# Value products as query x feature in a fused sink-window attention and two feed-forward layers

## The reference

```python
# q, k, v: 2 x 8 heads x 768 positions x 64, fp32
scores = q @ k.T / sqrt(64)
keep = (key < 4) | ((0 <= query - key) & (query - key < 128))
a = exp(where(keep, scores, -1e9) - rowmax)
a = a / (a.sum(-1) + 1e-9)
x = (a @ v)            # heads side by side: 1536 tokens x 512
h = x @ w_in;  x = max(0.01 * h, h) @ w_out        # 512 -> 2048 -> 512
h = x @ w_in2; y = (h * sigmoid(h)) @ w_out2       # 512 -> 2048 -> 512
```

## Time and profile before

| | us |
|---|---|
| median of three runs | 687.84 |
| the profiled execution | 690.34 |
| its span | 688.4 |
| PE busy | 634.6 |
| VectorE busy | 326.2 |
| ScalarE busy | 325.9 |
| GpSimd busy | 92.2 |

### The profile page before, as it was taken

How to read it: one execution, slowest core, us unless ns; L and a number is a source line. 1 busy time by engine, 2 the same in 40 slices (tenths; PEclk the granted TensorE clock), 3 DMA queues, 4 the chain that set the end, 5 groups by cost and what they waited for, 6 DMA issues and landing times.

```text
span 688.4 us, 9721 instructions
## 1 busy us (share of the span) xinstructions
PE 634.6 (92%) x3368; PEld 546.0 (79%) x3368; DVE 326.2 (47%) x780; ACT 325.9 (47%) x764; POOL 92.2 (13%) x117
## 2 busy tenths in 40 slices
PE   3649798979988999999999999999999999999997
PEld 3549798878887788888788888888888888888886
DVE  4786787746865666675322224333212322122321
ACT  5576677656765566664333336433323333223331
POOL 6341232222230322220000000000000000000000
PEclk9768999999999999999999999999999999999999
DMA  6643535413433213111002221323310112111001
GB/s 169 173 137 114 166 123 153 127 31 113 135 93 109 63 53 110 55 62 62 0 31 70 79 66 64 120 92 99 106 72 31 62 62 67 69 48 62 31 0 62
DMA packets 18096, 57.52 MB, mean 84 GB/s; under 512 B 2688, under 2 KB 2688, under 8 KB 18048
## 3 DMA queue, kind: packets, MB, share of 16 engines
q1 hardware_dynamic: 18048, 56.89, 26.9%
HBM read 53.74 MB, written 3.15 MB: 83 GB/s over the span
## 4 chain that ended last, share of the span: by engine, by line
PE 77%; DVE 10%; issue 5%; ACT 5%; DMA 1%; POOL 1%; SPq 0%; ACTq 0%; DVEq 0%; POOLq 0%
PE y_ps L841 34%; PE h_ps L810 33%; PE o_ps L774 3%; DVE sm L572 2%; PE y_ps L810 2%; PE t_ps L752 2%; PE s_ps L738 2%; DVE prob L646 2%; DVE x L593 1%; DMA qk_raw<-qk 1%; DVE win L599 1%; ACT pT L467 1%; DVE pT L582 1%; ACT q_st L447 1%; ACT win L479 1%
## 5 line engine op out<-in xcount | busy, mean ns | idle before, releaser
L810 PE MATMUL h_ps<-x,win 128*128 128x512 f32 (+1 forms) x1152 | 263.3, 374 | 6.1 <-DVE x L593 6.1
L810 PEld LDWEIGHTS h_ps<-x,win 128*128 128x128 f32 x1152 | 204.8, 190 | 42.4 <-issue 6.7
L610 DVE TENSOR_TENSOR g<-g_f,g 128x512 fp32r<-128x512 f32 (+1 forms) x112 | 72.4, 646 | 282.3 <-ACT g L494 282.3
L492 ACT ACTIVATE g_f<-h_ps 128x512 f32<-128x512 f32 (+1 forms) x96 | 53.9, 561 | 235.9 <-PE h_ps L810 235.6
L841 PE MATMUL y_ps<-g,wout 128*128 128x256 f32 (+1 forms) x768 | 153.6, 342 | 1.2 <-PE o_ps L774 0.9
L841 PE MATMUL y_ps<-wout,g 128*128 128x512 f32 x576 | 138.2, 389 | 0.0
L841 PEld LDWEIGHTS y_ps<-g,wout 128*128 128x128 f32 x768 | 120.9, 191 | 15.2 <-issue 1.5
L841 PEld LDWEIGHTS y_ps<-wout,g 128*128 128x128 f32 x576 | 108.1, 188 | 22.5
L436 ACT ACTIVATE prob<-sm,neg_max 128x260 f32<-128x260 f32 (+1 forms) x96 | 47.2, 491 | 65.5 <-DVE neg_max L572 64.8
L738 PE MATMUL s_ps<-k_hl,q_st 128*128 128x260 f32 (+1 forms) x162 | 35.8, 304 | 29.7 <-DVE neg_max L572 20.5
L599 DVE TENSOR_TENSOR win<-w_raw,win 128x512 fp32r<-128x512 f32 x72 | 53.5, 743 | 8.8 <-ACT win L479 8.4
(11 more groups left out here) (70 smaller groups left out, 428.0 us busy)
## 6 DMA issues: line engine op xcount, KB each, us to landing
w_raw<-w SPq DMA_DIRECT2D x72, 512.0 KB, 3.3
qk_raw<-qk SPq DMA_DIRECT2D x48, 260.0 KB, 4.7
v_raw<-vt SPq DMA_DIRECT2D x12, 256.0 KB, 2.6
y<-qk_raw SPq DMA_DIRECT2D x12, 256.0 KB, 2.2
vs_raw<-vsink SPq DMA_DIRECT2D x8, 8.0 KB, 2.3
```

The source lines that it names most:

```text
L492: nc.scalar.activation(g_f32[:, g_at(F)], h_of(F), func, alpha=slope)
L610: nc.vector.tensor_tensor(g[:, 1, g_at(F)], g_f32[:, g_at(F)], g[:, 0, g_at(F)].bitcast(F32), ALU.subtract).then_inc(g_ready, 1)
L810: ins = mm(h_of(F), win[:, split_slot[split_of[F]], wp, c * P:(c + 1) * P], x[:, xp, c, tokens(F)], start=(c == 0 and wp == HI and xp == H ...
```

## The change

- `weigh_values` swaps the operands: `pT` (128 keys x 128 queries of one head) is stationary and v moves with its 64 features. The result of a tile is query x feature for all 8 heads in one bank. `weigh_sinks` is one matmul of 512 columns for each tile.
- The probabilities are no longer scaled. `exp` collects the sums of a tile, `invert_sums` inverts 8 at a time, and a new `normalise(T)` multiplies the tile's result into `att` (128 x 512) in SBUF. Four transposes (job `"x"`) bring `att` to feature x query; `high` and `low` write it to `x`.
- `s_bank`: from slot 12 on the second score product of a slot gets a free bank of y (in slot 20, and from slot 36 on, `s_ps`), and stands behind the whole hidden step.
- `ticks_of`: two steps a slot for F = 0 to 13 (slots 11 to 17), then one. Step 32, the first wide one, moves from slot 35 to slot 36. The first two hidden steps move from the end of slot 10 into slot 11, behind the scores 22 and 23.
- ScalarE takes the hidden step ahead of the second exponential and the weight splits; the last transposes of tile T move into the middle of a hidden step in slot 4T + 6; SyncE issues the first two weight transfers before slot 0 and the next at slots 4 and 6; the sink values are stacked at slot 7 instead of 5; the zeroing of `prob_sink` is gone.

The matmul engine in a two-step slot: before, slot 13, `s_ps<-k_hl,q_st` are scores, `o_ps<-pT,v_hl` value products, `t_ps<-ident,prob` transposes.

The diff, cut to its core:

```diff
@@ the order
-    LAST = NPAIR + PAIRS
+    LAST = NPAIR + 4
-        n = (1, 1, 2)[(a - FS) % 3] if F < N_NARROW else 1
-        for _ in range(n):
+        for _ in range(2 if F < FT - 2 else 1):
-        lead = 0 if F == FT - 1 else 2 if F + 2 < N_NARROW else 1
+        lead = 2 if F + 2 < N_NARROW and F not in (FT - 2, FT - 1, FT) else 1
-    sinks_of = {2 * e + 3: e for e in range(NPAIR // 2) if has_sinks(e // 2)}
+    sinks_of = {PAIRS * T + 5: T for T in range(TILES) if has_sinks(T)}
+    x_of = {PAIRS * T + 6: T for T in range(TILES)}
@@ s_bank
+            a = n // 2
-            return (s_ps, y_ps[0], y_ps[1])[n % 3] if n < S_THREE else s_ps
+            if n < S_THREE:
+                return (s_ps, y_ps[0], y_ps[1])[n % 3]
+            if n % 2 == 0 or a == B1 or a >= B2:
+                return s_ps
+            return y_ps[2] if a < B1 else y_ps[0]
@@ sync
+            load_w(0)
+            load_w(1)
-                if 1 <= a <= RING:
-                    load_w(a - 1)
+                if a in (4, 6):
+                    load_w(a // 2)
@@ vector
-            def normalise(u):
-                W = width(u // PAIRS)
-                dve.wait_ge(exp_done, 2 * u + 2)
...
-                for i in range(2):
-                    a = prob[:, at + i, 0:W]
-                    nc.vector.tensor_scalar(a, a, row_inv[:, u % 2, 1, i:i + 1], None,
-                                            ALU.mult).then_inc(prob_ready, 1)
+            def invert_sums(T):
+                dve.wait_ge(exp_done, (T + 1) * H)
+                nc.vector.tensor_scalar_add(row_inv[:, 0, :], row_sum[:, T % 2, :], 1e-9).then_inc(norm_step, 1)
+                dve.wait_ge(norm_step, 2 * T + 1)
+                wait(dve, att_ready, T)
+                nc.vector.reciprocal(row_inv[:, 1, :], row_inv[:, 0, :]).then_inc(norm_step, 1)
+            def normalise(T):
+                dve.wait_ge(o_done, T + 1)
+                dve.wait_ge(norm_step, 2 * T + 2)
+                if T:
+                    dve.wait_ge(t_written, job["x", T - 1] + 1)
+                nc.vector.tensor_tensor(att[:, :].rearrange("p (h d) -> p h d", h=H),
+                                        o_bank(T)[:, :].rearrange("p (h d) -> p h d", h=H),
+                                        row_inv[:, 1, :].unsqueeze(2).to_broadcast([P, H, D]),
+                                        ALU.mult).then_inc(att_ready, 1)
@@ tensor
-                for s in slots:
-                    for vp, pp in PASSES:
-                        ins = mm(pair_out(u), v_hl[:, s, vp, p * P:(p + 1) * P],
-                                 pT[:, u % 2, pp, s * 2 * P:(s + 1) * 2 * P],
+                for i in range(2):
+                    h = 2 * p + i
+                    for s in slots:
+                        for pp, vp in PASSES:
+                            to = s * 2 * P + i * P
+                            ins = mm(o_bank(T)[:, h * D:(h + 1) * D], pT[:, u % 2, pp, to:to + P],
+                                     v_hl[:, s, vp, h * D:(h + 1) * D],
+                if a == FS:
+                    scores(2 * a + 1)
+                    for G in made_in[-1]:
+                        hidden(G, 0)
+                        hidden(G, 1)
                 for G in ahead[:1]:
                     hidden(G, 0)
-                if not head and a < NPAIR:
-                    scores(2 * a + 1)
+                if a in sinks_of:
+                    transposes("sinks", sinks_of[a])
+                if a in x_of and a <= NPAIR:
+                    transposes("pair", a - 1)
                 for n, G in enumerate(ahead):
                     if n:
                         hidden(G, 0)
                     hidden(G, 1)
+                if FS < a < NPAIR:
+                    scores(2 * a + 1)
```

More of the change, by code:

```diff
@@ L127, in sink_window_attention_two_ffn @@
             job["pair", a - 1] = len(job)
-    EARLY = next(a for a in range(LAST) if FT in ticks_of[a]) - 1
-    N_EARLY = job["pair", EARLY - 2] + 1
-    E_EARLY = 2 * NARROW // P
+        if a in x_of:
+            job["x", x_of[a]] = len(job)
+    N_EARLY = job["pair", FS - 2]
+    T_EARLY = NARROW // P
     S_FOUR, S_THREE = 2 * FS - 4, 2 * FS
+    B1, B2 = (next(a for a in range(LAST) if F in ticks_of[a]) for F in (FT, N_NARROW))
     with ExitStack() as ctx:
@@ L254, in width @@
             return P if T % TPB == 0 else PAN
[L256 to L260, removed]
         def j_split(T):
@@ L526, in _ @@
                     exp(2 * a)
-                    if head:
+                    if a <= FS:
                         exp(2 * a + 1)
-                if head and x_half is not None:
-                    high_x(x_half)
+                if a == FS:
+                    for G in made_in[-1]:
+                        take_hidden(G)
+                if a in sinks_of:
+                    high("sinks", sinks_of[a])
+                if not head and a in x_of and a <= NPAIR:
+                    high("pair", a - 1)
                 if head and j == j_split(T):
@@ L535, in _ @@
                 for n, F in enumerate([a - FS] if head else ticks_of[a]):
+                    evacuate(F - 1, 1)
+                    for G in made_in[F] if F >= 0 else ():
+                        take_hidden(G)
+                    if n == 0 and FS < a < NPAIR:
+                        exp(2 * a + 1)
                     for s in wout_in.get(F, ()):
                         high_wout(s)
[L538 to L540 removed]
                     for s in win_in.get(F, ()):
                         high_win(s)
[L543 to L546 removed]
                     evacuate(F, 0)
@@ L867, in _ @@
                     hidden(G, 1)
-                if a in sinks_of:
-                    transposes("sinks", sinks_of[a])
-                if head and 1 <= a:
-                    transposes("pair", a - 1)
-                if 2 <= a <= NPAIR + 1:
+                if FS < a < NPAIR:
+                    scores(2 * a + 1)
+                if a <= NPAIR + 1:
                     weigh_values(a - 2)
@@ L875, in _ @@
                     project(ticks[0], 0)
-                if not head and a <= NPAIR:
-                    transposes("pair", a - 1)
                 if a in sinks_of:
                     weigh_sinks(sinks_of[a])
+                if a not in x_of and a <= NPAIR:
+                    transposes("pair", a - 1)
+                if a in x_of:
+                    transposes("x", x_of[a])
                 if ticks:
                     project(ticks[0], 1)
-                if FT in ticks:
-                    for G in made_in[FT]:
-                        hidden(G, 0)
-                        hidden(G, 1)
                 for F in ticks[1:]:
```

184 lines of the change are left out of this document (86 added, 98 removed).

## The result

The changed kernel takes 705.15 us (median of 4 runs, 703.9 to 709.4) against 687.39 (686.6 to 688.4): a ratio of 1.027, 95% interval 1.022 to 1.032. It is slower by 2.7%, where 0.7% was forecast, and above the range. The profiled execution took 703.90 us with a span of 702.1; the one of before, 690.34 and 688.4. So the traces differ by 13.6 us and the medians by 17.8: the execution profiled before lay 3.0 us over this median (2.5 over the one of three runs), the one after 1.25 under. What follows is read from the traces.

What follows compares the result with a forecast made beforehand. The prediction took a ladder of matmul engine, VectorE and ScalarE to bound the middle, and matmul work the dense part. 23.5 - 1.6 - 3.4 - 13.8 = +4.7 us on 687.84 gave 692.5 us; likeliest range 689 to 698, wider 678 to 702.

Steps and rivals of the forecast that it cites:

- Part 1: Matmul engine: more value products at 0.109 us each, sink work and output transposes counted in, together +23.5 us.
- Rival B: Value products: the load of 64-column products hides, 30.6 us less, time 662; chance 0.05.
- Part 2: Behind the head: a shorter ladder of engines loses 25.0 us against 38.8, so -13.8 us.
- 23.5 - 1.6 - 13.8: Added matmul work, less 1.6 us of it moved ahead into the head, less 13.8 us from the shorter ladder.
- the 19.2 us of waits: Middle stretch: 14 waits of score products for the single score bank, claimed to disappear with a second bank.
- The clock's term: Middle stretch: 1.7 us still lost to the lower clock, a third of what it costs before.
- Part 3: The head, up to the first hidden step: -3.4 us, bounds -8 and +3.
- Two weight transfers leave the place in front of tile 2's queries: Head: tile 2's query split, which waited 4.96 us for a transfer, comes sooner; about 2.2 us gained.
- The trip of tile 1's output: Head: scaling, transposes, copy and subtraction take some 2.5 us in place of 1.3 for half a tile.
- VectorE's relief: Head: VectorE has 1.2 us less work per pair of heads.
- Rival D: Worse: gaps lower the clock more often (another 4 us), the head gains nothing (3.4); 700 us; chance 0.16 with beyond.
- The 705 us of the sentence behind the rivals: Some 705 us if waits for the score bank also stayed in part; called unlikely.

Runs made afterwards that it cites:

- b_noscale: The kernel before with the scaling of the probabilities left out, result not divided by the row sums: 675.97 us, 0.983.
- b_bank2: The kernel before with a second score bank for odd heads in both narrow blocks: 688.05 us, 1.0002.
- a_tbank: The changed kernel with its first narrow block back on one score bank and two transpose banks: 709.14 us, 1.031.
- a_stack5: The changed kernel with the sink values stacked in slot 5 again instead of slot 7: 709.28 us, 1.029.
- b_wearly: The kernel of b_recip with the change's order of weight transfers (two before the loop, next in slots 4 and 6): 680.26 us.
- a_tail: The changed kernel with sink values stacked in slot 5 and, for tile 1, output transposes and first hidden step moved earlier at the head's end: 702.09 us, 1.021.
- a_spread: The changed kernel with its seven two-step slots spread as every third slot over both narrow blocks: 708.74 us, 1.030.
- b_recip: The kernel before with a second score bank in the second narrow block only and no addition of 1e-9 to row sums: 680.45 us, 0.989.

## Why the prediction was wrong

The sign and the mechanism were right, the size was not. By the forecast's own steps:

- **Part 1, +23.5 us of PE work: right.** Its count of 1920 wide products is that of 80 wide steps, 32 to 111; the 95 in the description of the kernel before is wrong. 12 value products hold 1.26 us (1.31 forecast). Rival B, 64 columns for 0.040 us, is refuted by that row and by the 0.105 us that each product left out gave back. The sentence of the Trainium skill that would have made it cheaper still ("TensorE: Matmul & The Clock Gate", section "Back-to-back issue gap", some 60 cycles up to 64 columns) is for a product by itself; the same section says that in a stream of loads and products both set the spacing, and with that the trace agrees: 0.105 us, or 0.112 from 1.26 - 0.81 for four. (Its figure for such a stream of 128 columns, 81 ns, is below the 109 ns here, and the measurement decides.)
- **Part 2, -13.8 us: right.** From the first hidden step to the end of the span, the kernel after takes 645.5 us and before 636.5, +9.0; the forecast's terms for it are 23.5 - 1.6 - 13.8 = +8.1. VectorE's share in the ladder is confirmed by a run (b_noscale, -12.5 us in the narrow blocks), but the reason given was partly wrong: the second score bank by itself did not remove the 19.2 us of waits. In the first block it gave nothing (b_bank2, and a_tbank, where the waits sum up the same without it). VectorE's shorter work takes away 6.1 of them; that the second scores stand behind a whole hidden step is the likely cause of the rest, but no run has it alone. The clock's term (1.7 us still lost, a third of before) fits: from 63 to 204 us it was granted at 0.99 for 0.96.
- **Part 3, the head, -3.4 us: this is the step that failed.** It read +4.7, 8.1 us off and outside the forecast's own bounds of -8 and +3, and that is nearly all of the traces' miss of 8.9. Three things in it, together 6.7 us if 2.0 are put down to the transfers; the rest is open:
  - The stacking of the sink values was in the diff (slot 5 to slot 7) and not in the sum. It costs 3.1 us (a_stack5). On VectorE it runs just where its queue is the chain, and there GpSimd stretches it.
  - "Two weight transfers leave the place in front of tile 2's queries [...] that gives about 2.2." The split does come 2.5 us earlier (26.83 for 29.35), 0.9 of which is the late landing in the trace of before. In b_wearly it comes 0.7 earlier, and the head keeps at most 0.2. That the rest of the 2.5 was lost in the same way, to helpers whose queues end last, is argued and not shown.
  - The trip of tile 1's output was priced as VectorE's and ScalarE's work (2.5 us in place of 1.3), not as a place in line; and its twelve value products hold 2.77 us, for 2.4. It begins when pair 8's values are through and stands behind two scores and two masks: another order of the same work gives 1.6 us (a_tail). Only VectorE's relief was rightly seen: 1.1 to 2.0 us (b_noscale).
- **The medians.** The other 3.7 us of the miss lie between the executions profiled and the medians, in opposite directions. The forecast noted the first 2.5 and let it cancel.

Rival D came nearest to the head (nothing gained) and gave 700; it too expected no loss there. The 705 us of the sentence behind the rivals is met by luck: its condition, waits for the score bank that stay, did not hold.

## What to carry to other kernels

Before you credit the head of a kernel with a gain, find the engine whose queue is the chain there, and list every instruction that the diff moves on that engine, one-time set-up included. Small products cost what their weight load costs, so a layout that doubles their number is paid for at once wherever PE is dense; price that first. Where a ladder of engines sets the pace, look for its smallest operation: an addition of 1e-9 and its wait were worth 5.6 us. And before you credit an order of instructions with hiding waits, sum the waits and read the granted clock of both traces: a_spread, a_tbank and a_stack5 lost 4 to 8 us in the narrow blocks with no more waits than the kernel after.

## What was not expected of the hardware

- In the kernel after, the granted clock reads 1.00 from the start (the first change in its record stands at 61.3 us), while its products up to 56.6 us run at half pace: twelve value products take 2.77 us there and 1.26 later. In a_stack5 the record shows 0.50 from 40 to 58 us, with the same 2.77 us for the twelve. So ahead of the first change in a record, the pace of the products tells the clock and the record does not.
- Some VectorE operations take two to five times as long while GpSimd is at work, and others don't. Slowed are subtractions with both operands in SBUF and operations with a scalar: `win` L599 takes 1.78 us at 47.30, under GpSimd's subtractions that run from 46.91, and 0.69 at 42.69; the two-element addition 0.84 for 0.16. Not slowed are the reciprocal (0.15 to 0.17 us in b_recip, always) and operations that read PSUM: the pT subtraction takes 0.69 us either way in the trace of before. This agrees with the Trainium skill ("Trainium Architecture — The Big Picture", section "What this means for kernel authors"), which calls the port that the two share an exclusive lock. It is what makes a tiny operation dear, if it is of a kind that can be caught.
- Three runs of a_stack5 were 7 to 10 us above its fastest, and b_recip's four within 0.7 us. PE's falls to half pace in the narrow blocks go with it in the execution profiled; what sets them off stays open.
